# Linear attention and two feed-forward layers in fp32 on one core: the steps of all engines around the first layer in another order

## The reference

```
state = gamma[h]*state + k_t v_t^T ;  y_t = q_t state / 8        (per batch and head, over 768 positions)
x = y as 3072 tokens x 512
h = x @ w_in (512x1024) ; solu = h*softmax(h) ; x = layernorm(solu)*g_ln @ w_out (1024x512)
h = x @ w2_in (512x2048) ; out = (h*cos(h)) @ w2_out (2048x512)
```

## Time and profile before

| | us |
|---|---|
| median of three executions | 985.37 |
| the profiled execution, its device time | 981.93 |
| its span, first to last instruction | 980.1 |
| TensorE busy | 894.4 (91%) |
| VectorE, ScalarE, GpSimd busy | 617.1, 497.2, 209.9 |
| mean granted TensorE clock | 0.970 of full |

### The profile page before, as it was taken

One profiled execution on the slowest core, in us unless ns is written; L12 is line 12 of the kernel. 1 busy time (PEld: TensorE's weight loads), 2 busy tenths in 40 slices (PEclk: granted clock), 3 DMA queues, 4 the chain that ended last, 5 costly groups with the idle time before them and its releaser, 6 DMA issues.

```text
span 980.1 us, 14770 instructions
## 1 busy us (share of the span) xinstructions
PE 894.4 (91%) x5146; PEld 775.2 (79%) x5146; DVE 617.1 (63%) x864; ACT 497.2 (51%) x764; POOL 209.9 (21%) x238
## 2 busy tenths in 40 slices
PE   5759889899789888887799999999999999999998
PEld 5548667677668666776689999999999999999997
DVE  4885667666665766644465667566676557766554
ACT  1354544454444444446455556555664646655463
POOL 3752553444443455141000000000000000000000
PEclk8779999999999999998999999999999999999999
DMA  8433555445444643307297544563436544364401
GB/s 314 146 128 96 184 189 166 157 147 174 148 179 128 214 156 122 134 24 245 61 343 255 159 127 118 176 192 108 126 111 190 182 112 124 107 192 113 124 11 65
DMA packets 106664, 148.19 MB, mean 151 GB/s; under 512 B 7424, under 2 KB 77184, under 8 KB 106624
## 3 DMA queue, kind: packets, MB, share of 16 engines
q1 hardware_dynamic: 106624, 147.69, 46.7%
HBM read 112.01 MB, written 35.65 MB: 151 GB/s over the span
## 4 chain that ended last, share of the span: by engine, by line
PE 58%; issue 4%; POOL 2%; DVE 2%; ACT 1%; DMA 0%; POOLq 0%; ACTq 0%; DVEq 0%
PE bank L361 19%; PE bank L363 19%; PE bank L364 19%; POOL w_raw L1139 1%; PE bank L703 1%; PE bank L680 1%; DVE wo_out L1295 0%; PE bank L653 0%; PE bank L636 0%; POOL xs L1139 0%; DVE nmax L1251 0%; DVE z_l L1284 0%; PE bank L604 0%; ACT z_h L887 0%; POOL raw L1068 0%
## 5 line engine op out<-in xcount | busy, mean ns | idle before, releaser
L361 PE MATMUL bank<-yc_h,ring 128*128 128x384 f32 x448 | 152.5, 340 | 3.3 <-ACT c L1028 2.3
L363 PE MATMUL bank<-yc_l,ring 128*128 128x384 f32 x448 | 152.1, 340 | 0.0
L364 PE MATMUL bank<-yc_h,ring 128*128 128x384 f32 x448 | 151.7, 339 | 0.0
L361 PE MATMUL bank<-w1i_h,xv_h 128*128 128x512 f32 x168 | 73.8, 439 | 51.2 <-DVE work L1218 23.4
L1324 DVE SCALAR_TENSOR_TENSOR gg<-turns,c 128x768 f32<-128x768 int32 x64 | 61.0, 954 | 68.9 <-ACT turns L942 68.9
L361 PEld LDWEIGHTS bank<-yc_h,ring 128*128 128x128 f32 x448 | 84.6, 189 | 12.1 <-issue 4.7
L942 ACT ACTIVATE turns<-c 128x768 int32<-128x768 f32 x64 | 54.2, 846 | 78.3 <-DVE c L1394 75.8
L948 ACT ACTIVATE gg<-gg 128x768 f32<-128x768 f32 x64 | 54.1, 846 | 77.1 <-DVE gg L1331 77.0
L363 PEld LDWEIGHTS bank<-yc_l,ring 128*128 128x128 f32 x448 | 84.8, 189 | 7.0
L1139 POOL TENSOR_TENSOR y_raw<-y_raw,t 128x768 f32<-128x768 f32 x4 | 7.8, 1962 | 373.6 <-DVE yc_l L1306 373.6
L361 PEld LDWEIGHTS bank<-w1i_h,xv_h 128*128 128x128 f32 x168 | 33.3, 198 | 67.7 <-DVE work L1218 28.0
(11 more groups left out here) (121 smaller groups left out, 1957.6 us busy)
## 6 DMA issues: line engine op xcount, KB each, us to landing
ring<-w_split SPq DMA_DIRECT2D x224, 256.0 KB, 2.8
w_split<-w_out SPq DMA_DIRECT2D x16, 896.0 KB, 4.2
w2o_split<-wo_out SPq DMA_DIRECT2D x16, 512.0 KB, 4.6
w2o<-w2o_split SPq DMA_DIRECT2D x8, 1024.0 KB, 8.5
raw<-qT SPq DMA_DIRECT2D x24, 256.0 KB, 3.1
raw<-kT SPq DMA_DIRECT2D x24, 256.0 KB, 2.8
raw<-kn SPq DMA_DIRECT2D x24, 256.0 KB, 3.8
raw<-vn SPq DMA_DIRECT2D x24, 256.0 KB, 4.6
```

What stands on the lines that cost most here:

```text
L361: eng.matmul(dst, ah, bh, start=first and i == 0, stop=False, skip_group_check=read_between)
L363: eng.matmul(dst, ah, bl, start=False, stop=False, skip_group_check=read_between)
L364: m = eng.matmul(dst, al, bh, start=False, stop=last_one and i == n - 1, skip_group_check=read_between)
```

## The change

Two order lists change, and with them some steps:

- `STEP`: WH goes from the end of the iteration to behind EX (now ("WH", 1), the unit of the iteration before); WD and WE stand behind SM and before ST (both with 1); CEN goes from near the end to right behind U; XE goes behind ST.
- XH is split in XH (three of the five parts: A22, S1, S2) and XI (S3, S4), XL likewise in XL and XM, with XM last in the iteration. XS makes S1, S2, S3, S4 in that order (before: S1, S3, S2, S4). P6 and P7 wait for the half that they need.
- Filling: TS moves from GpSimd to VectorE and is taken apart in four; ScalarE does X before WVH; products P1, P2, P6, P5 of the first pair stand apart, with 30 dummy products of 128 columns (new step ZI) between; the first unit of w_out's rows is loaded into w1's first quarter (free once P1's low part and the first sum exist) in place of `c_b` (free only after P6's low part and all four sums), and its DMA is issued behind `load_next(1, 0)`, no longer ahead of it. WOH and WOL stand at other places of iterations 4 and 5; CEN(0) waits no longer for WOL.
- SyncE: `tile` calls `load_next` and `store_yt` first, then `swap_unit`; the wait for w1_in's passes before the first unit now stands in iteration 4 and also wants the first WOL.
- `late` and its keys are the same; since CEN moves within the iteration, what hangs on (26, "CEN") moves with it. The text of the new file holds a first version of `head`, `tail` and of the four lists that is overwritten by a second, equal one; the tail in it that is written out by hand has no effect.

```diff
-STEP = [("PK", 0), ("PV", 0), ("SG", 1), ("WE", 1), ("MO", 4), ("PA", 3), ("PC", 4), ("T0", 5),
-        ("PB", 3), ("PD", 4), ("ME", 4), ("T1", 5), ("EX", 4), ("OS", 1), ("SC", 0), ("DL", 1),
-        ("OP", 1), ("YT", 6), ("U", 4), ("SM", 0), ("X", 1), ("XE", 1), ("ST", 1), ("XS", 1),
-        ("WS", 0), ("L2a", 5), ("SQ", 4), ("XH", 1), ("L2b", 5), ("CEN", 4), ("XL", 1), ("VAR", 4),
-        ("WH", 0), ("WD", 0)]
+STEP = [("PK", 0), ("PV", 0), ("SG", 1), ("MO", 4), ("PA", 3), ("PC", 4), ("T0", 5), ("PB", 3),
+        ("PD", 4), ("ME", 4), ("T1", 5), ("EX", 4), ("WH", 1), ("OS", 1), ("SC", 0), ("DL", 1),
+        ("OP", 1), ("YT", 6), ("U", 4), ("CEN", 4), ("SM", 0), ("X", 1), ("WD", 1), ("WE", 1),
+        ("ST", 1), ("XE", 1), ("XS", 1), ("WS", 0), ("L2a", 5), ("SQ", 4), ("XH", 1), ("XI", 1),
+        ("L2b", 5), ("XL", 1), ("VAR", 4), ("XM", 1)]
...
-        q_out = [c_b, w1o_raw[:, 0, :], w1o_raw[:, 1, :], work[:, 2, :]]
+        q_out = [q11, two_rows(w1o_raw[:, 0, :]), two_rows(w1o_raw[:, 1, :]),
+                 two_rows(work[:, 2, :])]
...
-                    ("OS", 1), ("OP", 1), ("DL", 1), ("PA", 0), ("SC", 2), ("OS", 2), ("DL", 2),
-                    ("OP", 2), ("PB", 0), ("SC", 3)]
-        act_first = [("WVH", 0), ("X", 0), ("WVH", 1), ("X", 1), ("PA", 0), ("WVH", 2), ("XH", 1),
-                     ("WVH", 3), ("WVH", 4), ("X", 2), ("PB", 0), ("WVH", 5), ("WVH", 6)]
+                    ("OS", 1), ("OP", 1), ("DL", 1), ("ZI", 6), ("PA1", 0), ("ZI", 8), ("PA2", 0),
+                    ("SC", 2), ("OS", 2), ("DL", 2), ("OP", 2), ("PB1", 0), ("ZI", 4), ("PB2", 0),
+                    ("SC", 3), ("ZI", 12)]
+        act_first = [("X", 0), ("WVH", 0), ("X", 1), ("WVH", 1), ("WVH", 2), ("PA", 0), ("XH", 1),
+                     ("WVH", 3), ("XI", 1), ("X", 2), ("PB", 0), ("WVH", 4), ("WVH", 5),
+                     ("WVH", 6), ("WOH", 0)]
+        dve_first = [("QS", 0), ("ID", 0), ("SC0", 0), ("SC1", 0), ("QS", 1), ("ST", 0), ("XE", 0),
+                     ("SC0", 1), ("SC1", 1), ("TS", 0), ("WVL", 0), ("ST", 1), ("TS", 1),
+                     ("WVL", 1), ("WVL", 2), ("SC0", 2), ("SC1", 2), ("PA", 0), ("XL", 1),
+                     ("WVL", 3), ("ST", 2), ("TS", 2), ("XM", 1), ("WVL", 4), ("TS", 3),
+                     ("WVL", 5), ("WVL", 6), ("XE", 2), ("SC0", 3), ("SC1", 3)]
+        pool_first = [("NS", 0), ("NS", 1), ("SG", 1), ("XS", 1), ("QS", 2), ("NS", 2), ("SG", 2),
+                      ("QS", 3), ("NS", 3)]
...
-        outputs = {"U": 0, "ST": 1, "CEN": 2, "VAR": 3}
+        outputs = {(4, "EX"): [("WOH", 1)], (4, "SQ"): [("WOH", 2), ("WOH", 3)],
+                   (4, "XL"): [("WOL", 0)], (5, "PB"): [("WOL", 1)], (5, "T1"): [("WOL", 2)],
+                   (5, "CEN"): [("WOL", 3)]}
...
                     if u == KD:
-                        sp.wait_ge(w1i_lo, ORDER.index(P6) + 1)
-                        sp.wait_ge(ws_done, 4)
-                    sp.dma_start(two_rows(q_out[u - KD]), src).then_inc(ld_w1[u], 16)
+                        sp.wait_ge(w1i_lo, ORDER.index(P1) + 1)
+                        sp.wait_ge(ws_done, 1)
+                    sp.dma_start(q_out[u - KD], src).then_inc(ld_w1[u], 16)
...
+            load_next(1, 0)
             load_w1(KD)
-            load_next(1, 0)
...
             def tile(b, n):
-                swap_unit(b, n)
                 t = b * TILES + n
...
+                if isinstance(b, int) and t == 4:
+
+                    sp.wait_ge(w1i_lo, 7)
+                    sp.wait_ge(w1o_lo, 1)
+                swap_unit(b, n)
+
-            sp.wait_ge(w1i_lo, 7)
...
+                elif name == "ZI":
+
+                    pe.wait_ge(ident_done, 1)
+                    for _ in range(t):
+                        pe.matmul(ps_y[:, 0:128], ident[:, :], ident[:, :], start=True, stop=True)
...
                 elif p == P6:
-                    pair_wait(pe, xs_lo, b, m)
+                    pair_wait(pe, xs_lo, b, m, 2, 0)
...
                 elif p == P7:
+                    pair_wait(pe, xs_lo, b, m, 2, 1)
...
-                    pair_wait(act, xs_done, b, m, 4, 3)
-                    l1_wait(act, b, m - 1, P4)
-                    act.copy(xv_h[:, 2:7, :, :], xs[:, XA22:, :, :]).then_inc(xs_hi, 1)
+                    pair_wait(act, xs_done, b, m, 4, 1)
+                    l1_wait(act, b, m - 1, P4)
+                    act.copy(xv_h[:, 2:5, :, :], xs[:, XA22:XS2 + 1, :, :]).then_inc(xs_hi, 1)
+                elif name == "XI" and par == 1:
+                    pair_wait(act, xs_done, b, m, 4, 3)
+                    act.copy(xv_h[:, 5:7, :, :], xs[:, XS3:XS4 + 1, :, :]).then_inc(xs_hi, 1)
...
                 elif name == "CEN":
-                    if isinstance(b, int) and t == 0:
-                        dve.wait_ge(w1o_lo, 1)
```

More of the change, by code:

```diff
@@ L294, in build @@
                     head.append((name, n - behind))
-                if n == 4 and name in outputs:
-                    head += [("WOH", outputs[name]), ("WOL", outputs[name])]
+                head += outputs.get((n, name), [])
+        body = [(name, n - behind) for n in range(TILES) for name, behind in STEP]
+        for name, behind in STEP:
+            if behind and name not in ("WE", "WS", "WH", "WD"):
+                tail.append((name, NT - behind))
+        last = NT - 1
+        tail += [("MO", last - 2), ("PA", last - 1), ("T0", last - 3), ("PB", last - 1), ("TA", 0),
+                 ("T1", last - 3), ("EX", last - 2), ("U", last - 2), ("CEN", last - 2),
+                 ("SQ", last - 2), ("L2a", last - 3), ("YT", last - 4), ("L2b", last - 3),
+                 ("VAR", last - 2)]
@@ new lines, in build @@
+        tail += [("PC", last - 1), ("T0", last - 2), ("PD", last - 1), ("ME", last - 1),
+                 ("T1", last - 2), ("EX", last - 1), ("U", last - 1), ("CEN", last - 1),
+                 ("MO", last), ("SQ", last - 1), ("EX", last), ("YH", P1), ("YL", P1), ("U", last),
+                 ("L2a", last - 2), ("YH", P2), ("YL", P2), ("YT", last - 3), ("L2b", last - 2),
+                 ("SQ", last), ("VAR", last - 1), ("VAR", last), ("TBL", 0)]
+        tail += [("T0", last - 1), ("YH", P6), ("YL", P6), ("P", P1), ("P", P2), ("T1", last - 1),
+                 ("YH", P5), ("YL", P5), ("CEN", last), ("L2a", last - 1), ("YT", last - 2),
+                 ("P", P6), ("L2b", last - 1), ("YH", P3), ("YL", P3)]
@@ new lines, in build, with unit @@
+        tail += [("T0", last), ("P", P5), ("YH", P7), ("YL", P7), ("P", P3), ("T1", last),
+                 ("YH", P4), ("YL", P4), ("L2a", last), ("YT", last - 1), ("P", P7),
+                 ("L2b", last), ("P", P4), ("Q", P1), ("YT", last), ("Q", P2)]
+        def unit(b, n):
+            offset = n - (TILES - 2)
+            inside = n < TILES - 1 and (offset >= 0 or not isinstance(b, int) or b > 0)
+            return offset if inside and n >= 0 else None
+        head, tail = [], []
+        pe_first = [("Z", 11), ("SC", 0), ("Z", 4), ("OP", 0), ("DL", 0), ("Z", 2), ("SC", 1),
+                    ("OS", 1), ("OP", 1), ("DL", 1), ("ZI", 6), ("PA1", 0), ("ZI", 8), ("PA2", 0),
+                    ("SC", 2), ("OS", 2), ("DL", 2), ("OP", 2), ("PB1", 0), ("ZI", 4), ("PB2", 0),
+                    ("SC", 3), ("ZI", 12)]
@@ L297, in build @@
+        outputs = {(4, "EX"): [("WOH", 1)], (4, "SQ"): [("WOH", 2), ("WOH", 3)],
+                   (4, "XL"): [("WOL", 0)], (5, "PB"): [("WOL", 1)], (5, "T1"): [("WOL", 2)],
+                   (5, "CEN"): [("WOL", 3)]}
+        for n in range(4, TILES):
+            for name, behind in STEP:
+                if n >= behind:
+                    head.append((name, n - behind))
+                head += outputs.get((n, name), [])
         body = [(name, n - behind) for n in range(TILES) for name, behind in STEP]
@@ L657, in step @@
                     m.then_inc(o_done, 1)
-                elif name == "PA" and par == 0:
+                elif name in ("PA", "PA1") and par == 0:
                     l1(b, t, P1)
+                    if name == "PA":
+                        l1(b, t, P2)
+                elif name == "PA2":
                     l1(b, t, P2)
-                elif name == "PB" and par == 0:
+                elif name in ("PB", "PB1") and par == 0:
                     l1(b, t, P6)
+                    if name == "PB":
+                        l1(b, t, P5)
+                elif name == "PB2":
                     l1(b, t, P5)
@@ L834, in step @@
                     wait(act, o_done, b, t)
-                    pair_wait(act, xs_lo, b, m - 1)
+                    pair_wait(act, xs_lo, b, m - 1, 2, 1)
                     act.copy(xs[:, 2 * par:2 * par + 2, :, :].rearrange("p a k t -> p (a k) t"),
@@ L875, in step @@
                         k = 2 * t + n
-                        last = act.activation(w1o_h[:, k, :], q_out[t][:, n * 512:(n + 1) * 512],
+                        last = act.activation(w1o_h[:, k, :], q_out[t][:, n, :],
```

(1 more changed line is left out.)

54 lines of the change are left out of this document (29 added, 25 removed), and 8 rows, old and new, of the table dve_first.

## The result

The changed kernel took a median of 933.25 us (926.21 to 934.47, four runs), the one before 984.81 us beside it: ratio 0.947, 95% interval 0.942 to 0.953. Forecast were 937 us and a range of 919 to 966. The profiled execution was the fastest of the four: 926.2 us, span 924.4 of 980.1 us before.

A forecast was written before the change was run, and what follows sets the result against it. TensorE, the busiest engine, was held by waits for VectorE and ScalarE; steady state 32, filling 12 and change of halves 4.5 make 48.5 us off the median-scale 985.4: 937 us, range 919 to 966 (8 times in 10).

The forecast's parts named there:

- The removed waits: Steady state: TensorE's waits for h11 (20.4 us), h22 (13.1) and f1 (7.9) go, 41.4 us in all.
- Busy time beside them: Steady state: half-rate matmuls behind some stalls go too, 2 to 3 us, taken as 2.5.
- Given back (1), GpSimd's queue: Steady state: PK behind WS, which needs the later unit load, delays SC: 5 us lost (bounds 0 and 25).
- The sign that I gave: Steady state: a new wait of SC for GpSimd's scaling of q, under 1 us at each of six places.
- Given back (2), VectorE's line: Steady state, even iterations: WD and WE beside XS delay h11, 1 us at each of six pairs, 6 us lost.
- Filling: Start of the kernel: 12 us gained (4 to 17), with P4 of the first pair ending near 42 us.
- The clock sign: Filling: TensorE's granted clock would be above 0.78.
- Change of halves: Between the halves: T0(23)'s wait for CEN and most of T1(22)'s for z_l go, 4.5 us gained (0 to 7).
- (a): Rival, chance 0.15: GpSimd's queue is longer, 2.9 us more at each place, 32 us lost instead of 5; 964 us.
- (b): Rival, chance 0.17: VectorE and GpSimd lock each other, 12 us lost instead of 6, 3 more in the filling; 946 us.
- (c): Rival, chance 0.04: slower, every one of 12 iterations runs at the unit chain's own period; 998 us with a landing of 10.
- (d): Rival, chance 0.04: no gain, XL, XM and the maximum hold h11 as long, weights' loads bind the filling; 981 to 985 us.

The follow-up runs named there:

- border: The changed kernel with WH, WD, WE back at the border of the iterations and the unit's store and load back ahead of attention's loads: 980.6 us.
- passonly: The kernel before with only the move of WH, WD, WE and of the unit's store and load: 942.8 us.
- wslate: The changed kernel with WS moved from the end of iteration n to iteration n + 1, behind PK, PV and SG: 915.4 us.
- same: The changed kernel run again unaltered, as yardstick: 932.8 us, ratio 0.944 to 0.948 to the kernel before.
- fill: The changed kernel with WVH(4) ahead of X(2) on ScalarE, ZI 12 cut to 5 and the WOL passes placed earlier: 918.2 us.
- nozi: The changed kernel without the 30 dummy products: 931.0 us.
- cenback: The changed kernel with CEN back near the end of the iteration, behind L2b and ahead of XL, and the last WOL moved to U: 939.4 us.

## Why the prediction was right, point by point

- **The removed waits** (41.4 us: h11, h22, f1): all gone, shown by the profile after, by `border` (38.8 us come back) and by `passonly`.
- **Busy time beside them**: predicted 2.5 us, all of it half rate; measured 9.8 (busy 306.1 to 296.3 us), of which at most 5.2 at half rate. The other half I had put at nothing: at full clock too, each stall costs the overlap of the products on its two sides, some 0.3 us. This is the largest error of size. I counted one row; the view that sums it is the busy time over a stretch whose work doesn't change, and against the variant with no wait of SC (295.8) the kernel before had 10.3 us of it.
- **Given back (1), GpSimd's queue**: the right mechanism at the right place, predicted 5, measured 10.5 us. The term that was short is the landing: 4.3 us before, 5.6 after. The unit's load now follows four loads of attention, y's store and the store of the unit within 5 us; I had counted the issue times of that queue and not what it may do to the landing. All twelve profiled executions with this order have a median landing of 5.5 to 6.1 us, the two with the old one (before and `border`) 4.3; that the queue is the reason is argued, no run changes it alone. The sign that I gave, under 1 us at each of six places, was missed: SC waited at eight, up to 2.1 us. `wslate` shows the chain by taking PK out of it.
- **Given back (2), VectorE's line**: predicted 6, measured 0. No wait of P5 in the changed kernel; even without the split it is 1.6 us. The step that was wrong is the slack: I had h11 end within 0.2 us of P5's start, but it ends 0.9 us ahead of it, and VectorE itself waits for TensorE's product P2 there. VectorE's work in the pair was near what I said (24.6 us from 226.0 to 256.8).

```profile
254.33 0.69 DVE L1301 TENSOR_TENSOR work<-bank,f_a 128x512 f32<-128x512 f32 x1 [0.37 <-PE bank L421]
...
255.96 0.40 PE L418 MATMUL bank<-w1i_h,xv_h 128*128 128x512 f32 x1
```

- **Filling**: predicted 12, measured 7.5 (6.8 in `same`). P4 of the first pair ended at 46.5 us, not 42, 6.1 us sooner than before where 10.5 were predicted: ScalarE's X(2) waits for XM (10.1 us), WVH(4) behind it comes at 36.4 us and VectorE stands idle 3.3 us. I had worked out VectorE's line and not followed who holds ScalarE; `fill`, which changes this and other steps, ends P4 2.4 us sooner. And by `passonly` and `border` most of the stage's gain hangs on the passes' move, which I had counted for the steady state alone; so the lists of the filling gave less than the 7.5 us look like. The clock sign held (1.00 to 46.7 us, 0.78 before). The dummies take 0.25 us each, not 0.145: the row of before that I divided counts two records for each product. They are 7.5 us (the row below), not 4.4, but they cost nothing (`nozi`), since they lie in waits as was said.

```profile
0.00:50.00 50.00, 7.55 (x60) 7.16 (x60) 1.00 0.62 228
```

- **Change of halves**: predicted 4.5, measured 7.8. CEN's 3.2 us and 1.1 of z_l's 2.1 us went; `cenback` brings both waits back. The other 3.5 us lie in TensorE's busy time, which I had put at nothing here: 40.6 us at a granted clock of 0.90 before, 36.8 at 1.00 after, for the same work. First before, then after:

```profile
436.20:489.70 53.50, 40.64 (x191) 34.37 (x190) 26.57 (x43) 29.25 (x45) 3.75 (x5) 0.90 0.44 139
...
388.00:433.70 45.70, 36.80 (x192) 31.22 (x191) 28.00 (x43) 29.04 (x45) 4.39 (x5) 1.00 0.53 163
```

- **The sum**: 48.5 predicted, 51.6 between the medians (984.8 to 933.3). The errors have both signs: too little taken off for busy time and at the change of halves, too much given back on VectorE's line, and against them too little given back on GpSimd's queue and too much hoped of the filling. That the sum is near is in part luck. One slip besides: of the forecast's own bounds, 914 is on the scale of the profiled execution and 964 on that of the median; on the median's scale the lower one is 918.
- **The rivals**: (a) was right on the landing (5.6 us, it assumed 5.2) and wrong on the rest: the unit's four sums still took 1.82 us, not 2.9, and the stalls were 1.3 us each at eight places and not 3.6 and 1.8 at twelve. (b) came in part, but without its price. WE and XS do collide in the even iterations, at six places, where WE takes 1.22 to 1.23 us for 0.69; but WE took 1.52 at most places before, WD takes 1.08 us at all 16 places now, where it took up to 2.13 (in the odd iterations GpSimd stands idle for the load when WD runs), and P5 had the slack. The rows before and after fit the rule of the Trainium skill ("SBUF — State Buffer", Who interferes with whom) that the prediction names; what it would cost hung on the slack. (c) and (d) did not come.

## What to carry to other kernels

Work for which nobody waits must not stand, in any engine's fixed order, in front of a short operation for which the bound engine waits; here three such steps and a unit's DMAs were worth 44 of 987 us. When a step is moved past the issue of a load, follow the load's reader and what stands behind that reader on its queue: the new wait was there, and moving the reader one iteration later took it away for 17 us more. And price a stall as its length plus the busy time that it adds on its two sides, at half rate or not, read from the busy time of unchanged work.

## What the runs showed of the hardware that was not expected

- The busy time that went with short stalls was a quarter of what the stalls themselves cost: 9.8 us beside 41.4 us of waits, with single waits of at most 2.75 us. About half of it was half-rate time (granted clock 0.95 and 0.90 in two tenths of the stage, 1.00 elsewhere), the other half was lost overlap of products at full clock. SC's eight waits of 0.8 to 2.1 us left little of either (296.3 us busy against 295.8 without them), though in other executions of nearly the same order (`nozi`, `cenback`) the stage was busy 301 to 302 us at a clock of 0.98. What decides between these was not found.
- A load of 256 KB took 4.3 us to land when it followed one store, and 5.6 us when the same queue had been given six transfers within some 4 us before it (medians of 16; 5.5 to 6.1 in all kernels with that order). That the six are the reason was not tested alone.
- GpSimd's and VectorE's operations lengthened each other before (WD by up to 1.05 us, WE by 0.8). A change of order alone ended it for WD and left it at six of WE's 16 places (0.55 us each); GpSimd's busy time fell from 155.3 to 139.7 us in the steady state, and to 135.8 with WS moved.
